# Seven places in hand-written order lists of a fused attention, Strassen MLP and gated MLP kernel: sums, loads and products in other positions

## What is computed

```python
scores = scale * q @ k.T + alibi bias, masked to a causal window of 128   # 4 batches, 8 heads, 576 x 64
x = softmax(scores) @ v                                   # -> (4, 576, 512)
u = x + ((x.T @ U @ V)).T                                 # rank 32 mixing over the sequence
x = u + relu(u @ w_ch1) @ w_ch2                           # 512 -> 2048 -> 512
h = relu(x @ w_in); a, v = split(h)
v = (v - mean(v)) / sqrt(var(v) + 1e-6)
out = (a * (w_spatial @ v + b_spatial)) @ w_out
```

## Time and profile before

| what | us |
|---|---|
| median of 3 runs | 742.55 |
| lowest, highest | 742.05, 748.79 |
| the profiled execution, its own time | 744.08 |
| its span, first to last instruction | 742.3 |
| PE busy in it | 721.9 (97%) |
| DVE, ACT, POOL busy | 455.4, 339.3, 182.4 |

### The profile page before, as it was taken

How to read it: one execution, slowest core, us unless ns; L and a number is a source line. 1 busy time by engine, 2 the same in 40 slices (tenths; PEclk the granted TensorE clock), 3 DMA queues, 4 the chain that set the end, 5 groups by cost and what they waited for, 6 DMA issues and landing times.

```text
span 742.3 us, 13178 instructions
## 1 busy us (share of the span) xinstructions
PE 721.9 (97%) x4688; PEld 665.2 (90%) x4688; DVE 455.4 (61%) x1032; ACT 339.3 (46%) x764; POOL 182.4 (25%) x183
## 2 busy tenths in 40 slices
PE   8989999989999998999999999999999999999998
PEld 5767777779999998999899999999899998998997
DVE  6858686888855256325977965975466435444431
ACT  5967778855443234224344444444252432432422
POOL 1596645420005884326050000000010100100100
PEclk9999999999999999999999999999999999999999
DMA  6668875045465766797995354645940100100101
GB/s 205 187 236 308 293 261 175 16 142 170 150 216 199 286 245 220 281 346 296 422 304 192 117 167 148 216 163 166 357 167 1 49 17 0 64 0 0 64 0 64
DMA packets 74066, 128.24 MB, mean 173 GB/s; under 512 B 5024, under 2 KB 44960, under 8 KB 73504
## 3 DMA queue, kind: packets, MB, share of 16 engines
q1 hardware_dynamic: 74016, 127.59, 49.7%
HBM read 76.91 MB, written 50.66 MB: 172 GB/s over the span
## 4 chain that ended last, share of the span: by engine, by line
PE 79%; DVE 12%; issue 3%; POOL 2%; ACT 2%; DMA 1%; SPq 0%; DVEq 0%; ACTq 0%; POOLq 0%
PE bank L1862 7%; PE bank L1864 7%; PE bank L1863 7%; PE bank L1704 3%; PE bank L1904 3%; PE wide L1719 3%; PE bank L1905 3%; PE bank L1906 3%; PE bank L2013 2%; PE bank L2015 2%; PE bank L2014 2%; PE bank L1829 2%; PE bank L1827 2%; PE bank L1828 2%; DVE rk L1426 2%
## 5 line engine op out<-in xcount | busy, mean ns | idle before, releaser
L1862 PE MATMUL bank<-xs,w1s 128*128 128x384 f32 x336 | 113.9, 339 | 5.0 <-DVE tok L1416 2.3
L1863 PE MATMUL bank<-xs,w1s 128*128 128x384 f32 x336 | 113.1, 336 | 0.0
L1864 PE MATMUL bank<-xs,w1s 128*128 128x384 f32 x336 | 113.0, 336 | 0.0
L1045 ACT ACTIVATE rk<-tok 128x768 fp32r<-128x768 f32 x72 | 60.8, 848 | 77.5 <-PE bank L1906 34.2
L891 POOL TENSOR_TENSOR vl<-vr,vh 128x512 fp32r<-128x512 f32 x8 | 11.2, 1406 | 296.2 <-ACT vh L1169 296.2
L904 ACT ACTIVATE sc<-sc,mn 128x256 f32<-128x256 f32 (+1 forms) x144 | 67.0, 468 | 20.8 <-DVE mn L1229 20.6
L1028 ACT ACTIVATE sums_u<-bank 128x384 f32<-128x384 f32 x72 | 35.4, 491 | 89.6 <-PE bank L1864 89.3
L1904 PE MATMUL bank<-rk,w2q 128*128 128x384 f32 x208 | 70.6, 339 | 4.0 <-DVE rk L1426 3.0
L1862 PEld LDWEIGHTS bank<-xs,w1s 128*128 128x128 f32 x336 | 63.5, 189 | 7.4 <-DVE tok L1416 2.9
L1905 PE MATMUL bank<-rk,w2q 128*128 128x384 f32 x208 | 69.5, 334 | 0.0
L1906 PE MATMUL bank<-rk,w2q 128*128 128x384 f32 x208 | 69.5, 334 | 0.0
(11 more groups left out here) (220 smaller groups left out, 1850.5 us busy)
## 6 DMA issues: line engine op xcount, KB each, us to landing
r_scr<-tok SPq DMA_DIRECT2D x18, 768.0 KB, 4.2
tok<-r_scr SPq DMA_DIRECT2D x18, 768.0 KB, 6.0
qkraw<-qk SPq DMA_DIRECT2D x32, 288.0 KB, 3.9
w1raw<-w SPq DMA_DIRECT2D x32, 256.0 KB, 3.8
w2q<-w_scr SPq DMA_DIRECT2D x4, 2048.0 KB, 13.1
wc_scr<-wprep SPq DMA_DIRECT2D x12, 512.0 KB, 4.0
w_scr<-tok SPq DMA_DIRECT2D x11, 512.0 KB, 3.4
u_scr<-tok SPq DMA_DIRECT2D x6, 768.0 KB, 4.9
```

The costliest lines, as they stand in the source:

```text
L1045: act.activation(rk[:, n % RING, 0], raw[RAW_OF[m]][:, 2 * j:2 * j + 2, :], ACT.Relu if m <= 3 else ACT.Copy).then_inc(rk_hi, 1)
L1862: pe.matmul(o, wh, ah, start=(k == 0 and m in FRESH), stop=False, skip_group_check=True)
L1863: pe.matmul(o, wl, ah, start=False, stop=False, skip_group_check=True)
L1864: last = pe.matmul(o, wh, al, start=False, stop=(k == 1), skip_group_check=True)
```

## The change

It alters positions in lists and nothing in the arithmetic:

1. GpSimd's `w1_sum_1` comes at p = 3, behind `lo_x` and the splits of that pair, and no longer at p = 2.
2. `load_w1(2)` is issued in attention at p = 7.
3. The loads of the last two slices of the second weight matrix come one step later (s = 16 and 17).
4. The load of raw_c waits for product 7 of the last unit instead of product 3, and the stores and the next load keep their old wait behind it.
5. In the up phase DVE does `c22` of steps 7 and 15 ahead of `x_sum(g+1,4)` and `lo_xs(g+1,6)`; in steps 8 and 16 `lo_xs(g,4)` goes behind `c11` and `lo_xs(g,3)` behind `c22`.
6. The sums `r_sum` of each group have a list of their own, `SUMS`: group 0 begins one entry earlier; in group 1 the sums for product 4 come earlier; group 2 is new.
7. The last group's products go 6, 2, 7, 5 instead of 2, 6, 5, 7. The loads, stores and waits of SyncE and ACT that follow from it are exchanged accordingly (in the full diff: `load_u(2, 21)` ahead of `store_x2(2, 11)`, the first parts of the next phase's input in the order 2, then 0 and 1, and ACT's wait for product 2 instead of 6); the rule for `dc(g, 22)` is not touched.

```diff
+ORDER = {0: (2, 6, 5, 7), 1: (2, 6, 5, 7), 2: (6, 2, 7, 5)}
 for _g in range(G):
-    DN += [(_g, 1)] + ([(_g - 1, 3), (_g - 1, 4)] if _g else []) + [(_g, m) for m in (2, 6, 5, 7)]
+    DN += [(_g, 1)] + ([(_g - 1, 3), (_g - 1, 4)] if _g else []) + [(_g, m) for m in ORDER[_g]]
...
-W2_LOAD = {7: [0, 1], 9: [2], 10: [3], 11: [4], 12: [5], 15: [6], 16: [7]}
+W2_LOAD = {7: [0, 1], 9: [2], 10: [3], 11: [4], 12: [5], 16: [6], 17: [7]}
...
-FIRST_T = {(2, 1): [(3, 0), (2, 0)], (2, 2): [(3, 1), (2, 1)], (2, 3): [(3, 2), (2, 2)], (6, 0): [(3, 3), (2, 3)],
-           (6, 1): [(4, 0), (1, 0)], (6, 2): [(4, 1), (1, 1)], (6, 3): [(4, 2), (1, 2)], (5, 0): [(4, 3), (1, 3)]}
-NEXT_T = {(4, 1): [(3, 0)], (4, 2): [(3, 1)], (4, 3): [(3, 2), (2, 0)], (2, 0): [(3, 3), (2, 1)], (2, 1): [(2, 2)],
-          (2, 2): [(2, 3)], (2, 3): [(4, 0)], (6, 0): [(1, 0), (4, 1)], (6, 1): [(1, 1), (4, 2)],
-          (6, 2): [(1, 2), (4, 3)], (6, 3): [(1, 3)]}
+SUMS = {
+    0: {(2, 0): [(3, 0), (2, 0)], (2, 1): [(3, 1), (2, 1)], (2, 2): [(3, 2), (2, 2)], (2, 3): [(3, 3), (2, 3)],
+        (6, 0): [(4, 0), (1, 0)], (6, 1): [(4, 1), (1, 1)], (6, 2): [(4, 2), (1, 2)], (6, 3): [(4, 3), (1, 3)]},
+    1: {(4, 1): [(3, 0)], (4, 2): [(3, 1)], (4, 3): [(3, 2), (2, 0)], (2, 0): [(3, 3), (2, 1)],
+        (2, 1): [(2, 2), (4, 0)], (2, 2): [(2, 3)], (2, 3): [(4, 1), (4, 2)], (6, 0): [(1, 0), (4, 3)],
+        (6, 1): [(1, 1)], (6, 2): [(1, 2)], (6, 3): [(1, 3)]},
+    2: {(4, 1): [(3, 0), (2, 0)], (4, 2): [(3, 1)], (4, 3): [(2, 1), (3, 2)], (6, 0): [(2, 2), (3, 3)],
+        (6, 1): [(2, 3)], (2, 1): [(4, 0)], (2, 2): [(4, 1), (1, 0)], (2, 3): [(4, 2), (1, 1)],
+        (7, 0): [(4, 3), (1, 2)], (7, 1): [(1, 3)]}}
...
                 prepare(p)
+                if p == 7:
+                    load_w1(2)
...
             store_u(1, 1)
-            load_w1(2)
...
-            sp.wait_ge(up_p, UP_AT[(NU - 1, 3)])
+            sp.wait_ge(up_p, UP_AT[(NU - 1, 7)])
             sp.wait_ge(r_out[0], 16 * NU // 2)
             load_raw(0, "c", 0)
             load_raw(0, "c", 1)
             store_r(NU - 1)
+            sp.wait_ge(up_p, UP_AT[(NU - 1, 3)])
             load_w2q(5)
...
-                if p == 2:
+                if p == 3:
                     w1_sum_1()
...
                 if u == 0:
                     lo_xs(g, 5)
-                    lo_xs(g, 4)
...
                 c11(s)
+                if u == 0:
+                    lo_xs(g, 4)
                 if u == UNITS - 1 and g < G - 1:
                     lo_xs(g + 1, 2)
-                    x_sum(g + 1, 4)
-                    lo_xs(g + 1, 6)
...
+                c22(s)
                 if u == 0:
                     lo_xs(g, 3)
-                c22(s)
+                if u == UNITS - 1 and g < G - 1:
+                    x_sum(g + 1, 4)
+                    lo_xs(g + 1, 6)
...
-                for t, k in FIRST_T.get((m, j), []) if g == 0 and m != 4 else []:
-                    r_sum(0, t, k)
                 ahead = g + 1 if m == 4 else g
-                for t, k in NEXT_T.get((m, j), []) if 0 < ahead < G else []:
+                for t, k in SUMS[ahead].get((m, j), []) if ahead < G else []:
                     r_sum(ahead, t, k)
```

More of the change, by code:

```diff
@@ L653, in _ @@
                     load_group(range(0, WU))
-                store_x2(g, 11)
-                if g < G - 1:
+                if g == G - 1:
+                    load_u(g, 21)
+                    store_x2(g, 11)
+                else:
+                    store_x2(g, 11)
                     next_raw(g + 1, "a", 0)
-                load_u(g, 21)
-                if g < G - 1:
+                    load_u(g, 21)
                     next_raw(g + 1, "a", 1)
@@ L661, in _ @@
                     next_raw(g + 1, "b", 1)
-            sp.wait_ge(rk_lo, ENTRY[(G - 1, 5)] + DP)
+            sp.wait_ge(rk_lo, ENTRY[(G - 1, 7)] + DP)
             for n in x2_out:
                 sp.wait_ge(x2_out[n], 16 * (2 if n != 11 else 3))
+            load_x2(0, slice(2, 3), x2_first[1])
+            sp.wait_ge(rk_lo, ENTRY[(G - 1, 5)] + DP)
             load_x2(0, slice(0, 2), x2_first[0])
-            sp.wait_ge(rk_lo, ENTRY[(G - 1, 7)] + DP)
-            load_x2(0, slice(2, 3), x2_first[1])
             sp.wait_ge(rk_used, DN_AT[(G - 1, 5)])
@@ L673, in _ @@
             store_x2(G - 1, 21)
-            sp.wait_ge(rk_used, DN_AT[(G - 1, 7)])
             load_group(range(WO, WS))
@@ L1134, in _ @@
                 if g == G - 1 and j == 0 and m == 3:
-                    act.wait_ge(rk_used, DN_AT[(G - 1, 6)])
+                    act.wait_ge(rk_used, DN_AT[(G - 1, 2)])
                     hi_x2(0, [0, 1, 2])
```

## The result

The changed kernel takes 747.48 us (median of 22 runs, 746.01 to 749.05), the kernel before 742.93 (22 runs, 741.22 to 748.79): ratio 1.0051, 95% interval [1.0038, 1.0064]. It is slower by half a per cent, where 740.7 and a range up to 744.5 had been forecast. The profiled execution took 746.22 us with a span of 744.4.

What follows compares the result with a forecast made beforehand. PE, busy 97% of the span, was taken as the bound, so only its idle moments could be won, and DVE often had no free time. Nine terms summed to -1.8 us, from 742.55 to 740.7, range 736.5 to 744.5.

Steps and rivals of the forecast that it cites:

- step 4: Change to group 2: `c22` earlier ends product 3's stall, new 2.3 us stall at product 5, -1.0 us; later loads 0.
- step 5: Group 0 of the down phase: raw_c asked for 5 us earlier, but DVE sets the pace, -0.2 us.
- Steps 1 and 2: Attention: GpSimd's sums behind `lo_x`, -3.6 us including 1.67 of half clock; early `load_w1(2)` ends ACT's wait, -1.7 us.
- Rival D: Attention's gains don't arrive because another engine holds PE one step later: +1.8 us, 744.4; chance 0.04.
- Step 3: Change to group 1: `c22` earlier frees product 3 but holds PE longer at product 5, +0.7 us.
- Step 6: Group 1's sums in the down phase: low parts of entries (6,2) and (6,3) late, new stall elsewhere, +0.3 us.
- step 7: Group 2's new sums list in the down phase: low parts late in six stalls, +1.0 us.
- Step 8: Last group's order: product 4's old stall goes, but `dc(2, 22)` ahead of a low part stalls PE 2.15 us, +1.0 us.
- Step 9: The clock: one half-clock stretch counted for the new stalls at group 2's change and the last product 4, +1.7 us.
- rival B: DVE's new waits decide: half clock follows both new stalls, at group 2's change and last product 4; +1.5, 744.1; chance 0.12.

Runs made afterwards that it cites:

- attention alone: The kernel before with only places 1 and 2 of the change (GpSimd's sums one pair later, `load_w1(2)` in attention): 738.24 us, ratio 0.9916 to the kernel before.
- places 3 and 5 undone: The changed kernel without places 3 and 5, and with `dc(2,22)` moved to the last group's first entry of product 3: 739.57 us, ratio 0.9946 to the kernel before.
- the slice for product 6 late: The changed kernel with the 2 MB load `load_w2q(6)` issued behind raw_c: 744.62 us, ratio 1.002 to the kernel before.

## Why the prediction was wrong

**What failed: "They clear 287 to 292, where DVE is not urgent: 0"** (step 4, on the later loads of place 3) **and step 5's "raw_c can be asked for 5 us earlier".** The first looked only at whom the loads disturb where they were and are, not at what lies behind them in SyncE's list. The second counted the wait that the diff moved and not the one on the next line, for the store. In the kernel before that one was hidden, but only just. The last matmuls of product 7 and of product 3 of the last unit, and the issue rows of the store that raw_c waits for (the last number is the time from issue to landing), in this order before, attention alone, places 3 and 5 undone, and after:

```profile
336.02 0.33 PE L1864 MATMUL bank<-xs,w1s 128*128 128x384 f32 x1
...
346.42 0.33 PE L1864 MATMUL bank<-xs,w1s 128*128 128x384 f32 x1
```

```profile
r_scr<-late SPq DMA_DIRECT2D x1, 768.0 KB, 8.5
...
r_scr<-late SPq DMA_DIRECT2D x1, 768.0 KB, 8.8
...
r_scr<-late SPq DMA_DIRECT2D x1, 768.0 KB, 9.2
...
r_scr<-late SPq DMA_DIRECT2D x1, 768.0 KB, 11.3
```

Before, the store was issued at 337.37 and landed at 345.9; product 3 ended at 346.8 and raw_c was asked for at once. So there were 0.9 us of room, not 5. With attention's moves alone PE and the store come earlier together, and the room stays (0.5 us). The early request can't use more than this room, since product 7 is done before the store is even issued (336.35 and 337.37). The kernel with places 3 and 5 undone shows it: PE is where it is with attention alone, and raw_c is asked for 0.1 us earlier. First attention alone, then that kernel:

```profile
340.21 0.92 SPq L514 DMA_DIRECT2D raw_c<-r_scr  x2
```

```profile
340.09 0.92 SPq L519 DMA_DIRECT2D raw_c<-r_scr  x2
```

So place 4 gained nothing. With place 3's backlog the store needs 11.3 us, which nothing covers any more, and DVE comes to raw_c one entry sooner by the new list. Between 340 and 380 PE's stalls by distance were 3.9 us before and 8.9 after (1.5 of it half clock), +5.0 where step 5 had -0.2 with bounds to +0.3. The runs part it: place 3 costs 3.4 us in the changed kernel and 2.3 beside attention alone; group 0's list costs 2.3 with place 3 and 2.5, with group 1's, without it. The repairs add up: 3.4 (place 3), 3.6 (`dc(2,22)`), 0.8 (place 5) and 2.3 (group 0's list) one by one are 10.1 us, and the kernel with all four, and group 1's list, is 10.4 under the changed one.

**Steps 1 and 2** (-3.6, -1.7): right. The mixing product waits for nothing, PE restarts at 157.01 instead of 161.00 and is 5.3 to 5.7 us ahead behind attention, where 5.3 were forecast; the median of that kernel is 6.0 under before. Rival D is out.

**Steps 3 and 4**, the changes of group: the mechanism is right (no stall at product 3, a new one at product 5 at both), the sizes are a little off. Step 3 came to +0.9 (stalls of 1.68 and 0.27 us by distance where there were 0.69 and 0.32), forecast +0.7. At step 4's place the new stall is 1.87, forecast 2.3, beside two ahead of it that it hadn't (0.55 and 0.44). Without half clock, the stalls from 200 to 300 us sum to 5.8 us instead of 4.0. Step 4's gain of 1.0 leaned on the half clock of the earlier trace rows, which the timed runs don't all have; undoing place 5 gives back 0.8 us in the changed kernel.

**Step 6** (+0.3) and **step 7** (+1.0): right. Stalls of group 1 sum to 2.2 us against 1.9, those of group 2's sums to 2.9 against 1.8, in the entries that were named. **Step 8** (+1.0): right, 2.24 against 1.17 by distance, 2.15 forecast.

**Step 9**, the clock (+1.7): the clock loss is 4.0 us a run against 3.2, but by another path. Attention's moves took 2.3 us of it away (0.9 in that kernel), more than the 1.67 of step 1, and the new stalls of 2.92 and 2.24 us brought it back: moving `dc(2,22)` alone took off 2.0, undoing place 3 alone 2.7. In the one trace of the changed kernel only the first of them is followed by half clock; in three of the others that have the second, it is. One of these would have been near the forecast's stretch; both come in part of the runs, as rival B had it, though B put them at the change of group and the last product 4. The Trainium skill (TensorE: Matmul & The Clock Gate, What's actually happening) says that the monitor isn't reset at a kernel's start; the runs agree with what follows from it, since the 79 runs of one kernel go from 1.000, no such stretch, to 0.991 and once 0.989, the loss of four to five.

Put together at their measured sizes: -3.65 (attention's stalls) + 1.8 (changes of group) + 3.5 (start of the down phase without half clock) + 0.3 + 1.1 + 1.1 + 0.8 (clock) = +5.0, against 4.55 between the medians. That it comes so near is partly luck: the last term takes clock loss for lost time, and the runs at equal clock don't bear that out (at 0.998 the kernels are 3.6 us apart, at 0.993 2.0).

The stall of 1.53 us ahead of entry (0,1,3) went with place 3 too, by what looks like another path. The two low parts there took 2.90 us, where with place 3 undone they take 1.82. GpSimd's last splits of the second weight matrix, and the DMA share at that time, first in after (split, window), then with place 3 undone (split), then with the slice for product 6 late (window; columns as above):

```profile
342.87 1.28 POOL L829 TENSOR_TENSOR w2q<-w2raw,w2q 128x512 fp32r<-128x512 f32 x1
...
343.00:345.00 2.00, 0.65 (x4) 0.33 (x2) 2.00 (x2) 0.84 (x1) 1.14 (x1) 1.00 0.01 6
```

```profile
339.91 1.29 POOL L829 TENSOR_TENSOR w2q<-w2raw,w2q 128x512 fp32r<-128x512 f32 x1
```

```profile
343.00:345.00 2.00, 0.69 (x5) 0.37 (x4) 2.00 (x2) 0.84 (x1) 1.12 (x1) 1.00 1.06 387
```

The low parts take 2.90 us with the DMA engines idle (0.01) and 2.91 with them full (1.06), so transfers don't stretch them. The later slices make GpSimd end at 344.15 instead of 341.20, and the first low part falls into its last split. In the kernel with `dc(2,22)` moved they begin at 344.35, when GpSimd is done, and take 1.81. No experiment moves GpSimd's work alone, so this is read from traces and not shown by a run; and in the two kernels with place 3 and group 0's old list the low parts are stretched as well, yet the stall there is only 0.41 us.

What stays open is what a half-clock stretch costs where DVE sets the pace.

## What to carry to other kernels

A queue that only issues transfers has slack that no busy time shows. Before loads are moved later, or the engine in front is made faster, read for each wait in that queue how long its transfer had been landed when the wait was met (here 0.9 us), and look at the DMA share of the windows up to the next deadline: where it is 1.0, bytes put off now are paid at the end. An in-order engine should never have a wait for data that has just been asked for, or for what the bounding engine is just doing, ahead of the work which that engine needs next. Where clock stretches hang on stalls of about 2 us, count them over the timed runs and not in one profile.

## What the runs showed that was not expected

- A store of 768 KB landed in 4.2 us as the median of 18. The one ahead of raw_c took 8.5 us in the kernel before, behind a load of 2 MB that was issued 6.3 us ahead of it, 11.3 us in the changed kernel with the DMA share at 1.04, and 6.5 us there without the 2 MB. The rows of issues of the kernel before had a sign of it: its six late stores took 7.8 us (median).
- The same program loses from nothing to the clock of four half-clock stretches of 3.4 us and more: the kernel before 741.4 us at 1.000 and 742.8 at 0.998 (middle values of 13 and 18 runs). A stall of 1.94 us at the second change of group was followed by half clock in the profile of before and wasn't in that of attention alone.
- A lost clock is not always lost time: 3.7 us more of loss cost 2.7 us in the kernel before and 1.1 in the changed kernel.
- Two independent repairs of 3.4 and 3.6 us added up to 6.5. In both the stalls by distance shrank by less (2.4 and 2.24 us), and the clock loss fell as well (by 2.7 and 2.0).
